# Three moves in the attention phase of a retention and two-MoE kernel: a store to another queue, twelve subtractions to another engine, four loads to later steps

## The reference

```python
scores = q @ k.T / sqrt(64)                      # 8 batches, 8 heads, 576 tokens, head size 64
Dmat   = gamma[h] ** (i - j) if i >= j else 0    # gamma = 1 - 2 ** (-5 - h)
x = ((scores * Dmat) @ v) -> [4608, 512]
h = max(x @ w1, x @ w2, x @ w3)                  # 512 -> 768
x = h @ w_out                                    # 768 -> 512
g = ((x @ u1) * (x @ u2)) @ u3                   # 512 -> 1024 -> 1024
return g @ u_out                                 # 1024 -> 512
```

## Time and profile before

| | |
|---|---|
| median of 3 runs | 1258.05 us (1257.6 to 1260.22) |
| the profiled execution | 1256.95 us |
| its span in the profile | 1255.2 us |
| TensorE busy | 1224.5 us, 98% |
| VectorE / ScalarE / GpSimd busy | 63% / 39% / 33% |
| DMA, all through one ring of SyncE | 172.8 MB, 38.9% of 16 engines' span |

### The profile page before, as it was taken

The page is one execution under the profiler, slowest core; times in us unless marked ns, Lnnn a source line. Parts: engine busy times, 40 slices in busy tenths (PEclk is TensorE's granted clock), DMA queues, the critical chain, the costliest instruction groups (busy, mean ns, idle before and its releaser), DMA issues. The chain is left out here.

```text
span 1255.2 us, 21123 instructions
## 1 busy us (share of the span) xinstructions
PE 1224.5 (98%) x8288; PEld 1205.8 (96%) x8288; DVE 792.5 (63%) x1198; ACT 485.9 (39%) x771; POOL 409.0 (33%) x216
## 2 busy tenths in 40 slices
PE   7999999999999999999999999999999999899999
PEld 7899989999999999998999999999999999899998
DVE  6877747754646463668698767453545466867563
ACT  3343434423323232335554534242424243545441
POOL 2234319220202020063668561202020217266540
PEclk9999999999999999999999999999999999999999
DMA  9999944120202020143564441313132243444441
GB/s 365 347 362 355 352 141 163 37 91 32 95 26 101 26 96 32 52 151 120 180 206 169 160 151 51 108 51 101 56 103 90 81 163 107 151 151 152 157 158 64
DMA packets 87827, 174.15 MB, mean 139 GB/s; under 512 B 9648, under 2 KB 58416, under 8 KB 87728
## 3 DMA queue, kind: packets, MB, share of 16 engines
q1 hardware_dynamic: 87728, 172.80, 38.9%
HBM read 109.32 MB, written 63.44 MB: 138 GB/s over the span
## 5 line engine op out<-in xcount | busy, mean ns | idle before, releaser
L1033 PE MATMUL ps<-chi,whi 128*128 128x384 f32 x2016 | 676.0, 335 | 16.3 <-DVE wlo L760 7.6
L1035 PE MATMUL ps<-chi,wlo 128*128 128x384 f32 x2016 | 674.3, 334 | 0.0
L1034 PE MATMUL ps<-clo,whi 128*128 128x384 f32 x2016 | 674.1, 334 | 0.0
L551 POOL TENSOR_TENSOR raw<-raw,raw 128x768 f32<-128x768 f32 (+2 forms) x96 | 265.3, 2783 | 590.4 <-DMA raw<-xd 207.4
L1033 PEld LDWEIGHTS ps<-chi,whi 128*128 128x128 f32 x2016 | 378.9, 188 | 21.7 <-issue 10.3
L1034 PEld LDWEIGHTS ps<-clo,whi 128*128 128x128 f32 x2016 | 379.0, 188 | 0.0
L1035 PEld LDWEIGHTS ps<-chi,wlo 128*128 128x128 f32 x2016 | 378.8, 188 | 0.0
L760 DVE TENSOR_TENSOR clo<-raw,chi 128x768 fp32r<-128x768 f32 (+2 forms) x168 | 242.2, 1469 | 29.1 <-ACT chi L683 29.0
L683 ACT CAST chi<-raw 128x768 fp32r<-128x768 f32 (+2 forms) x168 | 180.2, 1080 | 86.3 <-PE ps L1035 58.7
L753 ACT COPY w<-ps 128x384 f32<-128x384 f32 x126 | 60.6, 481 | 228.8 <-PE ps L1035 227.3
L736 ACT COPY u<-ps 128x384 f32<-128x384 f32 x126 | 60.8, 483 | 174.4 <-PE ps L1035 173.0
(11 more groups left out here) (41 smaller groups left out, 845.9 us busy)
## 6 DMA issues: line engine op xcount, KB each, us to landing
qks<-qk SPq DMA_DIRECT2D x32, 576.0 KB, 6.6
gd<-h SPq DMA_DIRECT2D x96, 192.0 KB, 1.9
raw<-gd SPq DMA_DIRECT2D x24, 768.0 KB, 6.0
hd<-h SPq DMA_DIRECT2D x72, 192.0 KB, 1.9
raw<-hd SPq DMA_DIRECT2D x24, 576.0 KB, 5.8
vs<-vv SPq DMA_DIRECT2D x32, 320.0 KB, 7.7
raw<-xd SPq DMA_DIRECT2D x24, 384.0 KB, 5.1
x2d<-h SPq DMA_DIRECT2D x48, 192.0 KB, 2.1
```

The costliest lines, as they stand in the source:

```text
L551: return nc.gpsimd.tensor_tensor(out_, a, b, op)
L1033: nc.tensor.matmul(to, w1, x1, start=(start and k == 0), stop=False, skip_group_check=True)
L1034: nc.tensor.matmul(to, w1, x2, start=False, stop=False, skip_group_check=True)
L1035: last = nc.tensor.matmul(to, w2, x1, start=False, stop=(k == KH[st] - 1), skip_group_check=True)
```

## The change

1. `store_x` moves from SyncE's program to ScalarE's, directly behind `read_values(n)` of the same pair, so between the copies of the two pairs of a step.
2. `split_uo` and `split_u3`, the subtractions of the folding inputs, move from VectorE to the start of GpSimd's step.
3. The first two weights are loaded in steps 8 and 9 and not 4 and 5, and summed, cast and subtracted up to four steps later; the first token tile follows one step later.
4. At the start the last part of `dec` is loaded ahead of the values of pairs 2 and 3.

```diff
-P1_W_LOAD = {4: 0, 5: 1}
-P1_W_SUM = {5: (0, 0), 6: (0, 1), 7: (1, 0), 8: (1, 1)}
-P1_W_HI = {7: 0, 9: 1}
-P1_W_LO = {8: (0, 0), 9: (0, 1), 10: (1, 0), 11: (1, 1)}
-P1_RAW = 8
-P1_T = {9: 0, 10: 1, 11: 2, 12: 3}
-P1_HI = {11: 0, 12: 1, 13: 2, 14: 3}
-P1_LO = {12: 0, 13: 1, 14: 2, 15: 3}
+P1_W_LOAD = {8: 0, 9: 1}
+P1_W_SUM = {9: (0, 0), 10: (0, 1), 11: (1, 0), 12: (1, 1)}
+P1_W_HI = {11: 0, 13: 1}
+P1_W_LO = {12: (0, 0), 13: (0, 1), 14: (1, 0), 15: (1, 1)}
+P1_RAW = 9
+P1_T = {10: 0, 11: 1, 12: 2, 13: 3}
+P1_HI = {12: 0, 13: 1, 14: 2, 15: 3}
+P1_LO = {13: 0, 14: 1, 15: 2, 16: 3}
...
             load_qk(3)
+            load_decay(2, slice(4, HEADS))
             load_v(2)
             load_v(3)
-            load_decay(2, slice(4, HEADS))
...
                     if n + 4 < NP:
                         load_v(n + 4)
-                    if m:
-                        store_x(n - 2)
...
+            def split_uo(i):
+                pool.wait_ge(uo_hi, i + 1)
+                add(uolo[:, 2 * i:2 * i + 2, :], uoraw[:, 2 * i:2 * i + 2, :],
+                    uohi[:, 2 * i:2 * i + 2, :].bitcast(f32), ALU.subtract).then_inc(uo_lo, 1)
+
+            def split_u3(kb):
+                pool.wait_ge(u3_hi, kb + 1)
+                add(u3lo[kb % 2][:, :, :], u3raw[kb % 2][:, :, :], u3hi[kb % 2][:, :, :].bitcast(f32),
+                    ALU.subtract).then_inc(u3_lo, 1)
+
             for m in range(STEPS - 1):
+                if m in U3_SPLIT:
+                    split_u3(U3_SPLIT[m])
+                for i in UO_SPLIT.get(m, ()):
+                    split_uo(i)
...
+            def store_x(n):
+                b, p = divmod(n, PAIRS)
+                act.wait_ge(x_out, n + 1)
+                half = 3 * b // 2
+                cut = N if b % 2 == 0 else SEQ - N
+                for i, (lo, hi) in enumerate(((0, cut), (cut, SEQ))):
+                    to = 0 if (b % 2 == 0 or i == 1) else N - cut
+                    act.dma_start(acts[B][half + i, p // 2, :, p % 2, to:to + hi - lo], xst[:, n % 2, lo:hi]
+                                 ).then_inc(x_stored[n % 2], 16)
...
                 for n in read_in(m):
                     read_values(n)
+                    store_x(n)
```

More of the change, by code:

```diff
@@ L372, in load_uo @@
                 sp.dma_start(uoraw[:, 2 * i:2 * i + 2, :], uo[:, 2 * i:2 * i + 2, :]).then_inc(uo_loaded[i], 16)
[L374 to L382, removed]
             def load_u3(kb):
@@ L797, in make_state @@
                                 ALU.mult, ALU.add).then_inc(state_made, 1)
[L799 to L806, removed]
             def split_weight(wi, part):
@@ L831, in _ @@
                     decay_tail(n)
[L832 to L835, removed]
                 if m in P1_W_LO:
```

## The result

The changed kernel takes 1261.1 us in the median of 22 runs, the kernel before 1258.28 us in as many: ratio 1.0022, 95% interval 1.0013 to 1.003, so 2.8 us slower (1.6 to 3.8). The profiled execution took 1259.7 us, its span 1257.9 us, 2.7 us more than that of before.

What follows compares the result with a forecast made beforehand. TensorE, busy 98% of the span, bounds the kernel; only its gaps count. -3.87 - 1.23 - 0.28 + 8.06 + 0.3 = +2.98 us on a profiled 1256.95 us; predicted median 1261.0 us, range 1252 to 1266.5.

Steps and rivals of the forecast that it cites:

- rival 2: Issue at SyncE's cheap end, a pair 0.6 to 0.95 us: 1255.9 to 1260.4 us, no change to be measured; 25%.
- rival 4: Keys of step 9 come late, or SyncE and ScalarE hold each other up at issuing: 1262 to 1265 us; 8%.
- The issue between the copies: Two store issues on ScalarE delay its second copy: 0.62 us a step in steps 3 to 15, 8.06 us lost.
- The store's waits: ScalarE's copies into xst no longer wait for earlier stores in SyncE's ring: 3.87 us gained.
- the 2.19 us: Part of the loss in steps 3 to 10 put down to the stores, all taken as gained.
- `uolo`: Step 4: a pair of subtractions on VectorE held back state, probs and TensorE's query; moving them gains 1.23 us.
- Cost nothing: GpSimd, given the lower parts, delivers uolo and qdec in time, by 0.5 us at the least: no loss.
- The dec load: Step 1: the query's wait for probs, which first uses this table, goes: 0.28 us gained.
- the stores' 1.68: Scores of step 3 could start 1.68 us earlier without ScalarE's wait for a store.
- The tables: Later weight and token loads stand ahead of step 9's keys: costed at nothing, 1 to 3 us if the queue is long.
- signs of being wrong: Second copy 0.35 us behind the first, steps of 10.13 us, or new waits for qks, ks or uolo.
- The passage: Into stage B: copy s makes products 1.4 us later, an earlier weight load saves 1.1 us; net +0.3 us.

Runs made afterwards that it cites:

- the one with four issues: The changed kernel with each store cut into halves, four DMA issues a pair instead of two, same bytes: 1.0235 against the kernel before, 1288.4 us.
- the kernel with the last u3lo first: Changed kernel, stores behind both copies, old load tables, GpSimd's qdec ahead of u3lo from step 4 except step 15: 0.9977 against the kernel before, 1255.8 us.

## Why the prediction was right, and which of its terms were not

It said 1261.0 us, 0.24% slower; 1261.1 us and 0.22% were measured. The deciding mechanism, the issues that hold the second copy, is shown. That the number came within 0.1 us is luck: terms were off by up to 2 us, and they cancel. The pair of issues took 0.81 us, which is the condition of my rival 2 (0.6 to 0.95 us, "no change to be measured"): 13 x 0.37 = 4.8 us in place of 8.06 would have made the sum 1257.8 us. Two more losses brought it back, 1.4 us from dearer issues in crowded steps and 2.0 us from the keys, which rival 4 named at 8%.

- **The issue between the copies (8.06 us).** Right in kind, by the kernel with the stores behind both copies and by the one with four issues. Too large: a pair took 0.81 us where I took 1.0, and what else lay between the copies was 0.13 us where I had 0.18. A clean step lost 0.37 us and not 0.62. The crowded steps 5, 13 and 14, where the pair took 1.37, 1.33 and 0.96 us, lost 0.96, 0.89 and 0.51; steps 3 to 16 together 6.2 us (3.20 in steps 3 to 9, 0.37 in step 10, 2.18 in 11 to 14, 0.44 behind).
- **The store's waits (-3.87 us).** No copy of the changed kernel waits for a store (the two that the profile lists start 0.1 us behind an issue), so the 2.19 us are gone. With the store moved alone one wait remained, 1.69 us in step 3. No pair of runs isolates what the term is worth. My reason fell: nothing stands ahead of a store on ScalarE's ring, and it still lands after 6.4 us. What the rows show is an earlier issue. Before, a store could stand in SyncE's program behind value loads that were themselves slow to issue, here a copy of ScalarE that ends at 87.52 and its store:

```profile
86.88 0.64 ACT L642 COPY xst<-ps 128x576 f32<-128x576 f32 x1 [0.35 <-PE ps L981]
...
89.22 1.54 SPq L381 DMA_DIRECT2D xd<-xst  x2
```

The store went out 1.7 us later; on ScalarE it goes 0.03 us behind the copy (85.20, 85.23). With landings up to 9.3 us and 10.1 us between copies, 1.7 us can decide. That this is the whole reason is only argued; it fits that waits came back where the stores were issued behind both copies (9.4 us against none). The rule quoted from the Trainium skill, "DMA: Bandwidth & Descriptors", section "Issuing engines are not separate DMA queues", agrees with the landing times of this trace (6.4 us against 6.0). It does not follow that nothing is gained: the issue time that it calls usually small was the gain here, and on ScalarE the loss.
- **`uolo` (-1.23 us).** Step 4 is no longer than the others, 10.50 us. But "Cost nothing" for GpSimd was wrong: I followed the lower parts to TensorE and not `qdec` to SyncE's load, whose waits rose from 5.0 to 18.1 us. Alone the move gave nothing, and rather cost 2 us.
- **The dec load (-0.28 us).** Steps 1 and 2 together are 1.34 us shorter; with the stores' 1.68 I had 1.96. Step 1 gave 1.43 us, but not for my reason. The wait for `probs` that I had counted as gone rose from 0.28 to 0.88 us, and the scores before it took 2.45 us and not 4.48, because their matmuls ran faster (last section). Without that luck step 1 gives next to nothing: it took 9.97 us in the one kernel with the early load and slow matmuls. The load isn't idle, though: in the one with the late load and fast matmuls (the lower parts on GpSimd alone) TensorE waited 2.33 us for `probs` there. Step 2 then took the gain back in waits for keys of 1.12 and 0.37 us. I had not asked what an earlier TensorE would wait for next.
- **The tables (0).** The step that failed: "I cost it at nothing". A wait for `ks` that wasn't there before was also one of my signs of being wrong. SyncE's issues of step 9, the state sums of step 10, and the landing of all key loads:

```profile
98.72 0.49 SPq L377 DMA_DIRECT2D u3raw<-u3T  x1
...
100.37 2.84 SPq L416 DMA_DIRECT2D raw<-xd  x4
...
104.10 0.81 SPq L369 DMA_DIRECT2D ks<-kk  x2
...
115.68 1.33 PE L954 MATMUL ps<-vdec,ks 128*64 128x64 f32 x32 [1.68 <-issue]
...
DMA to landing us min/median/max: 2.9/5.0/11.7
```

The keys were issued at 104.1 behind 2.6 MB and landed up to 11.7 us later (8.3 at most before), 1.68 us late; step 10 took 12.49 us, 2.0 more than its neighbours. I had worked out 6.5 us of transfer ahead of them and a loss of 1 to 3 us if the queue were already long, and took the good case.
- **The passage (+0.3 us).** The products that wait for `s` start at 187.28, and the weight goes out right behind the last values:

```profile
187.28 0.45 PE L1033 MATMUL ps<-chi,whi 128*128 128x384 f32 x1 [1.54 <-ACT s L730]
...
184.53 0.34 SPq L410 DMA_DIRECT2D wraw<-wB  x1
```

They start 2.86 us behind the beginning of stage B and not 1.89 (182.91 - 181.02), 0.97 us later, and the wait for `w`, which I had put at 1.1 us (0.94 in its row), is gone: about nothing, and not +0.3.

Before stage B I had +2.68 us (-5.38 + 8.06) and 3.40 were measured: 1.9 us too much for the issues, 2.0 too little for the keys, 0.6 too much gain in steps 1 and 2. The rest of the span took 0.7 us less, which one execution can't tell from chance.

## What to carry to other kernels

A DMA issue between two instructions of ScalarE cost ScalarE its full issue time here; weigh the place between them, which holds the next instruction, against the place behind them, which makes the transfer later. When a DMA moves to another engine's program, price the issue time, and don't count on the other ring to land it sooner. When work moves to an idle engine, follow all that this engine releases, also the semaphores that a load waits for: in the changed kernel TensorE never waited for the moved subtractions, and the DMA issuer waited 18.1 us. And where a trace shows a long step, split it into gap and busy time before naming the cause: part of several here was the halved clock.

## What the runs showed of the hardware that I had not expected

A DMA issue on ScalarE takes as long as one on SyncE: 450 ns in the median, 326 at least, 1146 at most, against 433, 319 and 920.

A gap of TensorE can cost more than its length, as the granted clock fell to 0.50 in or behind gaps of 1.42 to 3.49 us in five of the profiled executions, and 1.2 to 3.0 us of busy time came on top. At that clock the 16 64x128 matmuls of a pair's scores took 2.08 us, 130 ns each, and not 1.16, here in the kernel with four issues:

```profile
171.84 2.08 PE L935 MATMUL ps<-qks 64*128 64x128 f32 x16 [2.46 <-ACT xst L644]
```

The same matmuls also took 2.08 us at the start of all 14 kernels, at about 4 and 9 us, and at about 13 us at one of the two speeds. The scores of pair 2 in the changed kernel, and in the kernel with the last u3lo first:

```profile
13.15 1.16 PE L933 MATMUL ps<-qks 64*128 64x128 f32 x16 [1.15 <-DVE probs L791]
```

```profile
13.20 2.08 PE L936 MATMUL ps<-qks 64*128 64x128 f32 x16 [0.97 <-DVE probs L794]
```

The granted clock is recorded as 1.00, the 2.4 GHz level, from 4 to 16 us in both, so in this stretch the record and the matmuls don't agree. Of the ten kernels with the early dec load, nine had the fast matmuls at 13 us; of the four with the late one, three had the slow ones. It makes most of the difference between a step 1 of 8.6 and of 10.0 us. The load's order can't be the only cause, and what is stays open.
